# A convolution tap moved to GpSimd in a fused attention and two-layer kernel, with two slots of the first layer moved ahead of the second

## The chip, the cores and the metric

The kernel runs on one core of a Trainium2 chip. The core has five engines, each with its own queue of instructions that runs strictly in order: TensorE (PE in the profile; its weight loads are shown apart as PEld), VectorE (DVE), ScalarE (ACT), GpSimd (POOL) and SyncE (SP), which here only issues DMAs. The engines meet at semaphores. The metric is the device time of one launch in microseconds (us), as the median of several runs.

## The reference

Three stages follow one another for 4 batches of 1088 tokens. Everything is float32.

```
# 1. attention with sketched features, 4 heads of 32
a, b = S1 @ x, S2 @ x                        # r = 8 each
phi(x) = outer(a, b)                         # 64 features
out = (phi(q) @ (phi(k).T @ v)) / (phi(q) @ sum(phi(k)) + 1e-6)

# 2. "layer 1": Fourier mixing, normalisation, an MLP (d_model 128, 512 hidden)
u  = x + real(fft(fft(x, tokens), channels))
un = (u - mean(u)) / sqrt(var(u) + 1e-6)
x2 = u + relu(un @ w_ch1) @ w_ch2

# 3. "layer 2": 1024 hidden channels, a convolution over tokens with 3 taps as gate
h    = relu(x2 @ w_in)
conv = w[0]*h[t-1] + w[1]*h[t] + w[2]*h[t+1]   # per channel
out  = (h * sigmoid(conv)) @ w_out
```

## The kernel before

All operands of a batch pair stay in the core's memory. The order of the work on every engine is written out by hand in one function per engine; nothing schedules it later.

**Attention** (the first 60 us or so) goes batch by batch: `sketches`, `key_values`, `feature_transposes` and `attend` on TensorE, copies out of PSUM on ScalarE, the features and the normalisation on VectorE. SyncE loads keys, queries and values; the queries of a batch come by one DMA (L280).

**Layer 1** is cut into 10 rounds `r` (two batch pairs by five token tiles) of four hidden chunks `c`. One pair (r, c) is a *slot*, numbered n = 4r + c, 0 to 41 (the last two only finish the work). All engines walk the slots in the same order. In a slot TensorE does `up(n)` and `down(n - 2)`. By the chunk, a slot also holds `token_sums(r + 3)` (c = 3) and `normed_transposes(r + 1)` (c = 1) on TensorE; `normed_rows`, `normed_high`, `mixed_high` on ScalarE; `mixed_rows(r + 2)`, `moments(r + 2)` (c = 1), `normed_low(r + 1)` (c = 2) and `mixed_low(r - 1)` on VectorE. The reciprocal standard deviations of a round are eight small instructions of 109x4 elements on GpSimd (L331 to L345), each waiting for the one before; before the change GpSimd does nothing else after its memsets, and they wait for `moments` (L887) alone.

**Layer 2** has 32 steps `i` (4 batches by 8 groups of 128 channels), each of 1088 tokens in three pieces. One step is: `hidden(i, t)` on TensorE (nine matmuls of 128x364, L458 to L460); `relu(i)` on ScalarE (L736, three pieces, into one of 5 buffers `h2`); `middle_tap(i)` on ScalarE (L744, `gate = w[1] * h2` into one of 7 buffers `gate`); `left_tap(i)` and `right_tap(i)` on VectorE (L957 and L962, each `gate += w * shifted h2`, two inputs from SBUF); `sigmoid(i)` on ScalarE (L749); `product(i)` on VectorE (L969, `gate *= h2`, two inputs from SBUF); `project(i)` on TensorE (L540). VectorE's own order in an iteration is `left_tap(i)`, slots, `product(i - 2)`, `right_tap(i)`, slots. ScalarE runs `relu(i + 1)` and `middle_tap(i + 1)`, slots, `sigmoid(i - 1)`.

The first `FIRST_SLOTS` = 22 slots run ahead of layer 2, since its first batches need round 4 finished; the other 20 are spread over the first 15 steps by `slots_a(i)` and `slots_b(i)`. From about step 14 on layer 2 is alone.

Of the kernel before, what the change touches and what calls it, by code (L numbers as in the profile page):

```python
# [89 lines left out]
def build(nc, kT_d, qT_d, v_d, s_d, ident_d, chan_d, cos_d, sin_d, w1_d, w2_d, win_d, wout_d, cw_d, out_d):  # L90
    with ExitStack() as ctx:
# [3 lines left out]
        def sem(name):  # L95
            return ctx.enter_context(nc.semaphore(name))
# [79 lines left out]
        ld_k, ld_q = [[sem(f"ld_{n}{i}") for i in range(2)] for n in "kq"]  # L176
        ld_first, ld_v, ones_ready = sem("ld_first"), sem("ld_v"), sem("ones_ready")
        ld_sketch, ld_ident, ld_tab, ld_w, ld_wout = (sem(n) for n in ("ld_sketch", "ld_ident", "ld_tab", "ld_w", "ld_wout"))
# [35 lines left out]
        def bank_h1(n):  # L214
            return 2 + n % 3 if n < FIRST_SLOTS else 2

# [17 lines left out]
        bank_of = {turn: 3 + n % 2 for n, turn in enumerate(tr_turns)}  # L234
        bank_of.update({turn: 5 + n % 3 for n, turn in enumerate(at_turns)})

        FIRST_SLOTS = NC1 // 2 + 2  # L240
        ALL_SLOTS = NC1 + 2
# [30 lines left out]
        def _(sp):  # L272
            def load_sketched(b):
                if b >= 2:
                    sp.wait_ge(sk_done, 4 * (b - 2) + 4)
                first = KQ_PIECES[0][2] * TK if b == 0 else 0
                if first:
                    sp.dma_start(kT[:, 0, 0:first], kT_d[:, 0, 0:first]).then_inc(ld_first, 16)
                sp.dma_start(kT[:, b % 2, first:], kT_d[:, b, first:]).then_inc(ld_k[b % 2], 16)
                sp.dma_start(qT[:, b % 2], qT_d[:, b, :]).then_inc(ld_q[b % 2], 16)  # L280

# [34 lines left out]
        def _(pool):  # L316
            pool.memset(kvz[:], 0.0).then_inc(kvz_zero, 1)
            pool.memset(half[:], -0.5).then_inc(half_set, 1)
            for x2 in (x2hi, x2lo):
                pool.memset(x2[:, :, 0:1].bitcast(F32), 0.0)  # L320
                pool.memset(x2[:, :, S + 1:SP].bitcast(F32), 0.0).then_inc(zeros_ready, 1)
            pool.wait_ge(half_set, 1)
            for r in range(NR):
                y = rstd[:, r % 2, :]
# [20 lines left out]
                pool.tensor_tensor(shift[:, r % 2, :], negmean, y, ALU.mult).then_inc(rstd_ready, 1)  # L345


        @block.tensor
        def _(pe):
# [10 lines left out]
            def sketches(b, pieces):  # L360

                for side, t0, t1 in pieces:
# [4 lines left out]
                    elif side == 0 and (t0 == 0 or b == 0):  # L367
                        pe.wait_ge(ld_k[b % 2], 16 * (b // 2 + 1))
                    if side == 1 and t0 == 0:
                        pe.wait_ge(ld_q[b % 2], 16 * (b // 2 + 1))  # L370
# [133 lines left out]
            def slot(n):  # L504
                r, c = divmod(n, C1)
                if n < NC1:
                    up(n)
                if 2 <= n < NC1 + 2:
                    down(n - 2)
                if c == 3 and r + 3 < NR:  # L510
                    token_sums(r + 3)
                if c == 1 and r + 1 < NR:
                    normed_transposes(r + 1)
# [53 lines left out]
            for n in range(TR_PIECES):  # L567
                features_and_values(B - 1, n)
                if n == 1:
                    token_sums(0)  # L570
                if n == 3:
                    token_sums(1)
# [12 lines left out]
            for n in range(2, FIRST_SLOTS):  # L585
                slot(n)
# [15 lines left out]
        def _(act):  # L602
# [13 lines left out]
            def feature_copies(b):  # L616
                for n in range(TR_PIECES):
                    act.wait_ge(tr_done, TR_PIECES * b + n + 1)
                    if b >= 1 and n == 0:
                        act.wait_ge(att_done, len(AT_PIECES) * b)  # L620
                    act.activation(qphiT[:, 4 * n:4 * n + 4, :].rearrange("p m t -> p (m t)"),
                                   ps[:, bank_of["features", b, n], 0:4 * TQ], ACT.Copy).then_inc(qphiT_ready, 1)
                    if b == B - 1 and n == 1:
                        sine_copy(0)
# [61 lines left out]
            def slot(n):  # L686
# [7 lines left out]
                if c == 1 and r >= 1:  # L694
                    mixed_high(r - 1)
                if c == 1 and r + 1 < NR:
                    normed_high(r + 1)
# [23 lines left out]
            sine_copy(2)  # L721
            slot(0)
            fold_copies(B - 1)
            slot(1)
            spectrum_copies(B - 1)

# [31 lines left out]

            for n in range(2, FIRST_SLOTS):
                slot(n)  # L760
            relu(0)
            middle_tap(0)
            for n in slots_b(0):
                slot(n)
            for i in range(NI + 1):
                if i + 1 < NI:
                    relu(i + 1)
                    middle_tap(i + 1)
                    for n in slots_b(i + 1):
                        slot(n)  # L770
# [9 lines left out]
        def _(dve):  # L780
# [131 lines left out]
            def slot(n):  # L912
# [38 lines left out]
            slot(0)  # L951
            slot(1)
            partner_fold(B - 1)

# [16 lines left out]

            for n in range(2, FIRST_SLOTS):
                slot(n)
# [108 lines left out]
```

## Time and profile before

| | |
|---|---|
| median of 3 runs | 276.6 us (275.37, 276.6, 279.46) |
| the profiled execution | 278.21 us, of which 276.4 us from the first to the last instruction (the span) |
| mean granted TensorE clock | 0.994 of full speed |
| instructions | 4299 |
| bytes moved by DMA | 13.04 MB |

The profile is of one execution. It has a page of summaries, and its trace answers further questions: the instructions of an engine in order of time (a timeline), groups of instructions of one line and shape with their mean duration, who waited for whom, the chain of work that ended last, and the busy time of each engine in a stretch. Times on a row are the start from the beginning of the span in us and the duration in us, unless ns is written. In square brackets stands the idle time ahead of an instruction, and what ended it. On VectorE and ScalarE an instruction's duration overlaps the next one's by a tenth of a microsecond or so; the distance from start to start is what one costs in a row of them.

### The profile page before, as it was taken

The numbers are of one execution on the slowest core, as the hardware profiler recorded it, in microseconds if no ns is written. First come the engines' busy times: TensorE is split into PE (matmuls) and PEld (weight loads), VectorE is DVE, ScalarE is ACT, GpSimd is POOL, SyncE is SP. The second block draws the span as 40 slices with busy tenths as digits, with TensorE's granted clock in tenths as the row PEclk, the third lists the DMA queues.
The fourth block names the chain that finished last, engine by engine and source line by source line (L and its number), as shares of the span: only waits on it lengthen the run. The fifth ranks groups of instructions, "written<-read, shape, count | busy, mean of one in ns | idle before, by whom it ended". The sixth has DMA issues, their size and how long they took to land.

```text
span 276.4 us, 4299 instructions
## 1 busy us (share of the span) xinstructions
PE 254.7 (92%) x1524; PEld 211.6 (77%) x1524; DVE 219.1 (79%) x384; ACT 186.5 (67%) x353; POOL 36.2 (13%) x90
## 2 busy tenths in 40 slices
PE   8799999989889999979887999999999999999955
PEld 7789999889778888868675777677677777777633
DVE  0746879877887677756686987958699999999993
ACT  2351426234466656648969889796999799999933
POOL 0000000003321233330270740000000000000000
PEclk9999999999999999979999999999999999999999
DMA  6859620200000000000000000000100010001002
GB/s 220 321 209 365 239 90 0 89 4 0 2 0 2 1 1 2 0 1 4 0 0 0 2 0 0 0 4 0 81 0 2 0 81 0 1 4 81 0 0 81
DMA packets 4197, 13.04 MB, mean 47 GB/s; under 512 B 720, under 2 KB 1488, under 8 KB 4176
## 3 DMA queue, kind: packets, MB, share of 16 engines
q1 hardware_dynamic: 4176, 12.77, 12.6%
q8 instruction: 12, 0.20, 0.3%
q14 instruction: 9, 0.07, 0.1%
HBM read 10.54 MB, written 2.23 MB: 46 GB/s over the span
## 4 chain that ended last, share of the span: by engine, by line
PE 45%; DVE 30%; ACT 15%; issue 5%; DMA 2%; POOL 1%; SPq 0%; ACTq 0%; DVEq 0%; POOLq 0%
DVE arena L969 8%; DVE arena L957 8%; DVE arena L962 8%; PE ps L540 7%; PE ps L458 5%; PE ps L451 5%; PE ps L375 5%; ACT arena L662 5%; PE ps L460 4%; PE ps L459 4%; PE ps L416 4%; PE ps L387 4%; ACT arena L749 3%; ACT arena L736 3%; DMA arena<-qT_d 2%
## 5 line engine op out<-in xcount | busy, mean ns | idle before, releaser
L540 PE MATMUL ps<-arena,wout 128*128 128x364 f32 (+1 forms) x192 | 63.8, 471 | 3.5 <-DVE arena L969 3.3
L540 PEld LDWEIGHTS ps<-arena,wout 128*128 128x128 f32 x192 | 35.5, 189 | 21.5 <-DVE arena L969 5.8
L957 DVE SCALAR_TENSOR_TENSOR arena<-arena,taps 128x1088 f32<-128x1088 f32 x32 | 43.5, 1359 | 6.4 <-ACT arena L744 6.4
L458 PE MATMUL ps<-x2hi,wlo 128*128 128x364 f32 x96 | 42.5, 442 | 5.9 <-ACT arena L736 4.2
L736 ACT ACTIVATE arena<-ps 128x364 f32<-128x364 f32 x96 | 40.6, 470 | 10.2 <-PE ps L460 9.9
L962 DVE SCALAR_TENSOR_TENSOR arena<-arena,taps 128x1088 f32<-128x1088 f32 x32 | 43.5, 1358 | 0.0
L969 DVE TENSOR_TENSOR arena<-arena 128x1088 f32<-128x1088 f32 (+2 forms) x36 | 41.8, 1176 | 1.5 <-ACT arena L749 1.5
L744 ACT ACTIVATE arena<-arena,taps 128x1088 f32<-128x1088 f32 x32 | 38.5, 1204 | 1.0
L749 ACT ACTIVATE arena<-arena 128x1088 f32<-128x1088 f32 x32 | 35.2, 1102 | 4.6 <-DVE arena L962 4.6
L460 PE MATMUL ps<-x2hi,whi 128*128 128x364 f32 x96 | 31.8, 332 | 0.0
L459 PE MATMUL ps<-x2lo,whi 128*128 128x364 f32 x96 | 31.7, 330 | 0.0
L458 PEld LDWEIGHTS ps<-x2hi,wlo 128*128 128x128 f32 x96 | 18.2, 189 | 15.1 <-ACT arena L736 9.8
L786 DVE TENSOR_TENSOR arena<-arena 121x2304 f32<-121x2304 f32 (+1 forms) x8 | 21.4, 2690 | 7.4 <-ACT arena L613 7.3
L613 ACT ACTIVATE arena<-ps 109x320 f32<-109x320 f32 (+2 forms) x16 | 6.8, 424 | 22.3 <-PE ps L375 21.2
L459 PEld LDWEIGHTS ps<-x2lo,whi 128*128 128x128 f32 x96 | 18.3, 190 | 4.1 <-issue 1.9
L901 DVE SCALAR_TENSOR_TENSOR h1lo<-ps,h1hi 128x436 fp32r<-128x436 f32 x22 | 13.3, 606 | 9.7 <-ACT h1hi L676 7.8
L331 POOL TENSOR_SCALAR arena<-arena 109x4 f32<-109x4 f32 x10 | 4.0, 401 | 121.5 <-DVE arena L887 121.5
L416 PE MATMUL ps<-arena 128*109 128x66 f32 x160 | 17.5, 261 | 1.3 <-DVE x_nat L826 0.6
L387 PE MATMUL ps<-arena 121*128 121x66 f32 x144 | 18.6, 270 | 0.0
L458 PE MATMUL ps<-unhi,wlo 128*128 128x436 f32 x40 | 17.4, 434 | 1.1 <-ACT arena L633 1.1
L375 PE MATMUL ps<-sketch,arena 128*109 128x64 f32 (+1 forms) x152 | 16.9, 264 | 1.4 <-DMA arena<-qT_d 1.4
L460 PEld LDWEIGHTS ps<-x2hi,whi 128*128 128x128 f32 x96 | 18.2, 190 | 0.0
(81 smaller groups left out, 441.3 us busy)
## 6 DMA issues: line engine op xcount, KB each, us to landing
arena<-v_d SPq DMA_DIRECT2D x4, 594.0 KB, 4.2
arena<-qT_d SPq DMA_DIRECT2D x4, 545.0 KB, 7.0
arena<-kT_d SPq DMA_DIRECT2D x3, 544.5 KB, 7.0
out_d<-arena SPq DMA_DIRECT2D x3, 544.0 KB, 2.7
cos_t<-cos_d SPq DMA_DIRECT2D x1, 926.5 KB, 5.6
sin_t<-sin_d SPq DMA_DIRECT2D x1, 926.5 KB, 7.4
wraw<-w_d SPq DMA_DIRECT2D x2, 256.0 KB, 5.0
wraw<-win_d SPq DMA_DIRECT2D x1, 512.0 KB, 5.9
```

The source lines that it names most:

```text
L375: mm = pe.matmul(ps[0:rows, bank_kq(n), c:c + H * AB], src[:, b % 2, t * rows:(t + 1) * rows], sketch[:], start=True, stop=True)
L387: mm = pe.matmul(ps[:, KV_BANK, pair * 2 * V1:(pair + 1) * 2 * V1], kphi[:, b % 2, t, 2 * pair:2 * pair + 2, :].rearrange("p h f -> p (h f)"),
L458: pe.matmul(out, lo, rhi, start=first, stop=False)
L459: pe.matmul(out, hi, rlo, start=False, stop=False)
L460: return pe.matmul(out, hi, rhi, start=False, stop=last)
L540: pe.matmul(ps[:, OUT_BANK + t, 0:z - a], wout[:, c, :], gate[:, i % GATES, a:z], start=(c == 0), stop=(c == C2 - 1)).then_inc(wout_done, 1)
L736: act.activation(h2[:, i % HIDDENS, t * TT:(t + 1) * TT], ps[:, bank_p(n), 0:TT], ACT.Relu).then_inc(h2_ready, 1)
L744: act.activation(gate[:, i % GATES, 1:S + 1], h2[:, i % HIDDENS, 1:S + 1], ACT.Copy, scale=taps[:, i % C2, 1:2]).then_inc(mid_ready, 1)
L749: act.activation(gate[:, i % GATES, 1:S + 1], gate[:, i % GATES, 1:S + 1], ACT.Sigmoid).then_inc(gate_ready, 1)
L957: dve.scalar_tensor_tensor(out=gate[:, i % GATES, 1:S + 1], in0=h2[:, i % HIDDENS, 0:S], scalar=taps[:, i % C2, 0:1], in1=gate[:, i % GATE ...
L962: dve.scalar_tensor_tensor(out=gate[:, i % GATES, 1:S + 1], in0=h2[:, i % HIDDENS, 2:S + 2], scalar=taps[:, i % C2, 2:3], in1=gate[:, i % ...
L969: dve.tensor_tensor(gate[:, i % GATES, a:z], h2[:, i % HIDDENS, a:z], gate[:, i % GATES, a:z], ALU.mult).then_inc(prod_ready, 1)
```

## The change

`middle_tap` moves from ScalarE to GpSimd, as a `tensor_scalar` with a per-channel multiplier. GpSimd's loop over the rounds is split up so that it walks the slots like the other engines: `reciprocal_deviations(r + 2)` stands in slot c = 1 of round r, behind the middle taps of the steps before it in the queue and ahead of those after it.

Two more slots (22 and 23) run ahead of layer 2: `FIRST_SLOTS` is 24. Around the last batch of attention, slot 1 comes before `fold_transposes(B - 1)` and slot 2 before its spectra; token sums 0 come one piece later; inside a slot, `normed_transposes` and `normed_high` move from c = 1 to c = 2, `normed_low` from c = 2 to c = 3, and the early `mixed_low` from c = 3 to c = 2. The bank of PSUM for two turns changes with it. The first queries are loaded by two DMAs of half the size, and the first query sketches wait for the first of them alone.

The core of the diff:

```diff
-        FIRST_SLOTS = NC1 // 2 + 2
+        FIRST_SLOTS = NC1 // 2 + 4
...
-                sp.dma_start(qT[:, b % 2], qT_d[:, b, :]).then_inc(ld_q[b % 2], 16)
+                part = KQ_PIECES[2][2] * TQ if b == 0 else 0
+                if part:
+                    sp.dma_start(qT[:, 0, 0:part], qT_d[:, 0, 0:part]).then_inc(ld_half, 16)
+                sp.dma_start(qT[:, b % 2, part:], qT_d[:, b, part:]).then_inc(ld_q[b % 2], 16)
...
+            def middle_tap(i):
+                pool.wait_ge(h2_ready, NT * (i + 1))
+                if i >= GATES:
+                    pool.wait_ge(wout_done, NT * (i - GATES + 1))
+                pool.tensor_scalar(gate[:, i % GATES, 1:S + 1], h2[:, i % HIDDENS, 1:S + 1], taps[:, i % C2, 1:2], None,
+                                   ALU.mult).then_inc(mid_ready, 1)
+
+            def slot(n):
+                r, c = divmod(n, C1)
+                if c == 1 and r + 2 < NR:
+                    reciprocal_deviations(r + 2)
+
+            pool.wait_ge(half_set, 1)
+            reciprocal_deviations(0)
+            reciprocal_deviations(1)
+            for n in (*range(FIRST_SLOTS), *slots_a(0), *slots_b(0)):
+                slot(n)
+            pool.wait_ge(ld_wout, 32)
+            for i in range(NI):
+                middle_tap(i)
+                for n in (*slots_a(i + 1), *slots_b(i + 1)):
+                    slot(n)
...
-                if c == 1 and r + 1 < NR:
+                if c == 2 and r + 1 < NR:
                     normed_transposes(r + 1)
...
-                if n == 1:
+                if n == 2:
                     token_sums(0)
...
             slot(0)
+            slot(1)
             fold_transposes(B - 1)
-            slot(1)
+            slot(2)
             channel_spectra(B - 1)
...
-            def middle_tap(i):
-                act.wait_ge(h2_ready, NT * (i + 1))
-                if i == 0:
-                    act.wait_ge(ld_wout, 32)
-                if i >= GATES:
-                    act.wait_ge(wout_done, NT * (i - GATES + 1))
-                act.activation(gate[:, i % GATES, 1:S + 1], h2[:, i % HIDDENS, 1:S + 1], ACT.Copy,
-                               scale=taps[:, i % C2, 1:2]).then_inc(mid_ready, 1)
...
-                if c == 2 and r + 1 < NR:
+                if c == 2 and 1 <= r < NJ:
+                    mixed_low(r - 1)
+                if c == 3 and r + 1 < NR:
                     normed_low(r + 1)
-                if c == 3 and 1 <= r < NJ:
-                    mixed_low(r - 1)
```

On GpSimd the end of the queue before is the last of ten such groups of eight:

```order
L331 TENSOR_SCALAR arena<-arena 109x4
L333 TENSOR_TENSOR arena<-arena,half 109x4
L334 TENSOR_SCALAR arena<-arena 109x4
L337 TENSOR_TENSOR arena<-arena 109x4
L339 TENSOR_TENSOR arena<-arena 109x4
L341 TENSOR_SCALAR arena<-arena 109x4
L343 TENSOR_TENSOR arena<-arena 109x4
L345 TENSOR_TENSOR arena<-arena 109x4
```

On GpSimd the end of the queue in the change, from the last instruction of round 8's group (L350) on; L356 is the middle tap, and the group between is round 9's:

```order
L350 TENSOR_TENSOR arena<-arena 109x4
L356 TENSOR_SCALAR arena<-arena,taps 128x1088 x4
L336 TENSOR_SCALAR arena<-arena 109x4
L338 TENSOR_TENSOR arena<-arena,half 109x4
L339 TENSOR_SCALAR arena<-arena 109x4
L342 TENSOR_TENSOR arena<-arena 109x4
L344 TENSOR_TENSOR arena<-arena 109x4
L346 TENSOR_SCALAR arena<-arena 109x4
L348 TENSOR_TENSOR arena<-arena 109x4
L350 TENSOR_TENSOR arena<-arena 109x4
L356 TENSOR_SCALAR arena<-arena,taps 128x1088 x28
```

So all of round 8's group now stands ahead of the first middle tap, and round 9's between the fourth and the fifth.

On VectorE before, where layer 2 begins (L957 left tap, L962 right tap; L866 and L872 `mixed_rows`, L881 and L887 `moments`, L894 `normed_low`, L908 `mixed_low`):

```order
L887 BN_AGGR arena<-arena 109x2 x4
L894 TENSOR_TENSOR unlo<-ps,unhi 128x436
L957 SCALAR_TENSOR_TENSOR arena<-arena,taps 128x1088
L962 SCALAR_TENSOR_TENSOR arena<-arena,taps 128x1088
L866 TENSOR_TENSOR arena<-ps,arena 109x130 x2
L872 TENSOR_TENSOR arena<-x_nat,arena 109x2x64 x4
L957 SCALAR_TENSOR_TENSOR arena<-arena,taps 128x1088
L908 TENSOR_TENSOR x2lo<-ps,x2hi 128x2x109
L908 TENSOR_TENSOR x2lo<-ps,x2hi 128x2x108
L881 BN_STATS arena<-arena 109x6 x4
L887 BN_AGGR arena<-arena 109x2 x4
```

On VectorE in the change, the same place (L979 left tap, L984 right tap; L887 and L893 `mixed_rows`, L902 and L908 `moments`, L915 `normed_low`, L929 `mixed_low`):

```order
L915 TENSOR_TENSOR unlo<-ps,unhi 128x436
L887 TENSOR_TENSOR arena<-ps,arena 109x130 x2
L893 TENSOR_TENSOR arena<-x_nat,arena 109x2x64 x4
L929 TENSOR_TENSOR x2lo<-ps,x2hi 128x2x109
L929 TENSOR_TENSOR x2lo<-ps,x2hi 128x2x108
L902 BN_STATS arena<-arena 109x6 x4
L908 BN_AGGR arena<-arena 109x2 x4
L979 SCALAR_TENSOR_TENSOR arena<-arena,taps 128x1088
L984 SCALAR_TENSOR_TENSOR arena<-arena,taps 128x1088
L979 SCALAR_TENSOR_TENSOR arena<-arena,taps 128x1088
L984 SCALAR_TENSOR_TENSOR arena<-arena,taps 128x1088
```

`mixed_rows(8)`, a `mixed_low` and `moments(8)` have moved from behind the first left tap to ahead of it.

## Rows read from the trace of the kernel before

**Rows 1.** The page, busy time and share of the span by engine.

```profile
PE 254.7 (92%) x1524; PEld 211.6 (77%) x1524; DVE 219.1 (79%) x384; ACT 186.5 (67%) x353; POOL 36.2 (13%) x90
```

**Rows 2.** Windows of all engines: stretch, length, busy us (instructions) each, PE clock, DMA.

```profile
126.46:201.79 75.33, 70.80 (x324) 52.31 (x323) 60.21 (x81) 64.67 (x118) 15.87 (x16) 1.00 0.02 8
201.79:265.29 63.50, 61.56 (x265) 46.73 (x266) 63.50 (x53) 58.60 (x90) 0.00 (x0) 1.00 0.05 18
260.00:264.00 4.00, 2.31 (x8) 1.06 (x6) 4.00 (x5) 3.34 (x6) 0.00 (x0) 1.00 0.00 0
120.00:122.00 2.00, 2.00 (x8) 1.95 (x7) 1.01 (x6) 0.94 (x2) 1.28 (x3) 0.54 0.00 0
```

**Rows 3.** The chain of work that ended last, in order of time: start, us, what.

```profile
98.74 1.33 PE ps L451 x12
...
106.21 1.33 PE ps L451 x12
...
265.29 1.26 DVE arena L957
266.56 1.21 DVE arena L969
267.81 5.79 PE ps L540 x18
```

**Rows 4.** Timeline of VectorE, 126 to 163 us.

```profile
126.46 1.35 DVE L957 SCALAR_TENSOR_TENSOR arena<-arena,taps 128x1088 f32<-128x1088 f32 x1 [5.42 <-ACT arena L744]
...
158.41 1.34 DVE L962 SCALAR_TENSOR_TENSOR arena<-arena,taps 128x1088 f32<-128x1088 f32 x1
159.67 1.34 DVE L957 SCALAR_TENSOR_TENSOR arena<-arena,taps 128x1088 f32<-128x1088 f32 x1
160.93 1.28 DVE L969 TENSOR_TENSOR arena<-arena 128x1088 f32<-128x1088 f32 x1
162.13 1.35 DVE L962 SCALAR_TENSOR_TENSOR arena<-arena,taps 128x1088 f32<-128x1088 f32 x1
```

**Rows 5.** Timeline of GpSimd, 60 to 170 us: an undisturbed group's ends, then one in layer 2.

```profile
112.58 0.20 POOL L331 TENSOR_SCALAR arena<-arena 109x4 f32<-109x4 f32 x1 [4.64 <-DVE arena L887]
...
115.20 0.20 POOL L345 TENSOR_TENSOR arena<-arena 109x4 f32<-109x4 f32 x1
...
153.15 1.14 POOL L331 TENSOR_SCALAR arena<-arena 109x4 f32<-109x4 f32 x1 [9.31 <-DVE arena L887]
...
158.62 1.19 POOL L343 TENSOR_TENSOR arena<-arena 109x4 f32<-109x4 f32 x1
159.89 2.39 POOL L345 TENSOR_TENSOR arena<-arena 109x4 f32<-109x4 f32 x1
```

**Rows 6.** Groups by line and shape, whole span: count | busy us, mean ns | idle before.

```profile
L744 ACT ACTIVATE arena<-arena,taps 128x1088 f32<-128x1088 f32 x32 | 38.5, 1204 | 1.0
L317 POOL MEMSET arena<- 128x132 f32 x1 | 0.2, 208 | 0.3 <-POOLq L1074 0.3
L320 POOL MEMSET x2hi<- 128x4 f32 x1 | 0.1, 105 | 0.0
```

**Rows 7.** Waits: who for whom, us in total, times, longest us.

```profile
DVE x2lo L908 <- ACT x2hi L682: 12.5, 5, 3.0
PE ps L471 <- ACT arena L662: 2.4, 6, 0.5
PE ps L375 <- DMA arena<-qT_d: 1.4, 1, 1.4
PE ps L458 <- DVE x2lo L908: 1.4, 1, 1.4
```

**Rows 8.** Timeline of TensorE and ScalarE where layer 2 begins.

```profile
119.71 0.41 PE L458 MATMUL ps<-x2hi,wlo 128*128 128x364 f32 x1 [1.36 <-DVE x2lo L908]
...
125.14 1.21 ACT L744 ACTIVATE arena<-arena,taps 128x1088 f32<-128x1088 f32 x1
```

More of the change, by code:

```diff
@@ L176, in build @@
         ld_k, ld_q = [[sem(f"ld_{n}{i}") for i in range(2)] for n in "kq"]
-        ld_first, ld_v, ones_ready = sem("ld_first"), sem("ld_v"), sem("ones_ready")
+        ld_first, ld_half, ld_v, ones_ready = (sem(n) for n in ("ld_first", "ld_half", "ld_v", "ones_ready"))
         ld_sketch, ld_ident, ld_tab, ld_w, ld_wout = (sem(n) for n in ("ld_sketch", "ld_ident", "ld_tab", "ld_w", "ld_wout"))
@@ L214, in bank_h1 @@
         def bank_h1(n):
-            return 2 + n % 3 if n < FIRST_SLOTS else 2
+            return 2 + n % 3 if n < NC1 // 2 + 2 else 2
         def bank_x2(r):
@@ L235, in build @@
         bank_of.update({turn: 5 + n % 3 for n, turn in enumerate(at_turns)})
-        FIRST_SLOTS = NC1 // 2 + 2
+        for n in range(2):
+            bank_of["folded", B - 1, n] = bank_of["spectra", B - 1, n] = (5, 7)[n]
+        FIRST_SLOTS = NC1 // 2 + 4
         ALL_SLOTS = NC1 + 2
@@ L321, in _, with reciprocal_deviations @@
                 pool.memset(x2[:, :, S + 1:SP].bitcast(F32), 0.0).then_inc(zeros_ready, 1)
-            pool.wait_ge(half_set, 1)
-            for r in range(NR):
+            def reciprocal_deviations(r):
                 y = rstd[:, r % 2, :]
@@ L368, in sketches @@
                         pe.wait_ge(ld_k[b % 2], 16 * (b // 2 + 1))
-                    if side == 1 and t0 == 0:
+                    if side == 1 and t0 == 0 and b == 0:
+                        pe.wait_ge(ld_half, 16)
+                    elif side == 1:
                         pe.wait_ge(ld_q[b % 2], 16 * (b // 2 + 1))
@@ L581, in _ @@
             slot(0)
+            slot(1)
             fold_transposes(B - 1)
-            slot(1)
+            slot(2)
             channel_spectra(B - 1)
-            for n in range(2, FIRST_SLOTS):
+            for n in range(3, FIRST_SLOTS):
                 slot(n)
@@ L622, in feature_copies @@
                                    ps[:, bank_of["features", b, n], 0:4 * TQ], ACT.Copy).then_inc(qphiT_ready, 1)
-                    if b == B - 1 and n == 1:
+                    if b == B - 1 and n == 2:
                         sine_copy(0)
@@ L695, in slot @@
                     mixed_high(r - 1)
-                if c == 1 and r + 1 < NR:
+                if c == 2 and r + 1 < NR:
                     normed_high(r + 1)
@@ L722, in _ @@
             slot(0)
+            slot(1)
             fold_copies(B - 1)
-            slot(1)
+            slot(2)
             spectrum_copies(B - 1)
@@ L757, in output @@
                     act.activation(outT[:, b % 2, a:z], ps[:, OUT_BANK + t, 0:z - a], ACT.Copy).then_inc(out_ready, 1)
-            for n in range(2, FIRST_SLOTS):
+            for n in range(3, FIRST_SLOTS):
                 slot(n)
             relu(0)
-            middle_tap(0)
             for n in slots_b(0):
@@ L767, in _ @@
                     relu(i + 1)
-                    middle_tap(i + 1)
                     for n in slots_b(i + 1):
@@ L952, in _ @@
             slot(1)
+            slot(2)
             partner_fold(B - 1)
@@ L970, in product @@
                                       ALU.mult).then_inc(prod_ready, 1)
-            for n in range(2, FIRST_SLOTS):
+            for n in range(3, FIRST_SLOTS):
                 slot(n)
```

## The prediction

> **What bounds the kernel now.** I read the busy shares first, then the chain of waits, then windows cut at the steps of layer 2. The page alone misleads: TensorE is busy 92% of the span and VectorE 79% [rows 1], which looks like a kernel bound by TensorE. The windows say where each engine limits. Between left taps 14 and 31 (201.79 to 265.29 us) VectorE is busy 63.50 of 63.50 us [rows 2]: 17 steps at 63.50 / 17 = 3.735 us. That is 1.26 us from start to start of a left tap, 1.20 of a product, 1.26 of a right tap [rows 4], and nothing between them. ScalarE is busy 58.60 us there and does not set the pace [rows 2]. Between left taps 0 and 14 (126.46 to 201.79 us), where 20 slots of layer 1 are mixed in, VectorE is busy 60.21 of 75.33 us and TensorE 70.80 [rows 2]; of VectorE's 15.1 us of idle time most is the five waits of `mixed_low` for ScalarE, 12.5 us [rows 7], behind TensorE's slots. The rest of the span after left tap 31 is 276.4 - 265.29 = 11.1 us of product, projection and store [rows 3].
>
> So layer 2 is VectorE's own chain for its second half and close to it in the first. The middle tap costs ScalarE 32 x 1.204 us = 38.5 us [rows 6], and none of that is on VectorE's path in the second half. Taking it from ScalarE can give back something only in the first half, or before it.
>
> **GpSimd beside VectorE.** The question is what a GpSimd instruction of 1088 columns does beside VectorE's taps. The trace has no such instruction, but it has small ones in both surroundings. Round 7's group of eight, with VectorE on PSUM work or idle, runs from 112.58 to 115.40 us, 2.8 us, single instructions at 0.20 us [rows 5]. Round 9's begins at 153.15 and ends at 162.28 us, 9.1 us for the same eight [rows 5]. Its members last until a tap or product of VectorE ends: L343 ends at 159.81, right tap L962 at 159.75; L345 starts at 159.89, lasts through left tap L957 (to 161.01) and product L969 (to 162.21), and ends at 162.28 [rows 4, 5]. So a GpSimd instruction does not run while VectorE runs an instruction with two inputs from SBUF, and once it even missed the change-over. The Trainium skill ("SBUF — State Buffer", who interferes with whom) has this as a rule: the two engines share a pair of ports, held by one of them for a whole instruction, and a VectorE instruction with two SBUF inputs needs it against a GpSimd one that reads SBUF. The trace agrees as far as GpSimd waiting for VectorE goes; that VectorE waits for GpSimd in turn no row shows, since 0.2 us fits into a change-over (VectorE's starts keep their 1.26 us) [rows 4]. All three VectorE instructions of a step are of the kind that kept GpSimd out, and they fill the engine. A long GpSimd instruction therefore must either hold VectorE off, or wait until VectorE runs dry for want of the next middle tap. Either way the two take turns.
>
> **How long the tap is on GpSimd.** The lower bound: two memsets, 132 columns in 208 ns and 4 in 105 ns, give 103 / 128 = 0.80 ns a column [rows 6]; with 0.20 us for a small instruction [rows 5], 0.20 + 1084 x 0.80 = 1.07 us. The upper bound: reading and writing cost that slope each, 0.20 + 1084 x 1.61 = 1.94 us. I take 1.1 us, since the memset is the only row with a slope and ScalarE does the same thing in 1.20 [rows 6]. The Trainium skill ("GPSIMD Engine Reference", engine selection) puts one-input elementwise work on GpSimd at roughly line rate, and advises VectorE for such work; no run here has shown it yet, and the sum would be the same by it.
>
> **The sum,** against the execution's own span of 276.4 us.
>
> 1. *Second half of layer 2.* In turns, a step costs 3.735 + 1.1 + about 0.1 for the hand-over and the semaphore = 4.95 us. 17 x (4.95 - 3.735) = +20.7 us. The path is then left tap, product, right tap, middle tap of the next step. ScalarE (less its 1.2 us a step) and TensorE, busy at most 61.56 / 17 = 3.6 us a step, are clear of it [rows 2].
> 2. *First half.* VectorE's busy 60.21 us [rows 2] lose some 3.6 us, as one `mixed_rows`, one `mixed_low` and one `moments` now stand ahead of left tap 0: 56.6. Fourteen middle taps at 1.2 us add 16.8: 73.4. Round 9's group stands between middle taps 3 and 4: VectorE gets no left tap 4 until the group (2.8 us undisturbed, longer beside product 1 and right tap 3) and then the tap are through, about 3 us of VectorE idle. Of the 15.1 us of idle time before, most was VectorE waiting for TensorE's slots; a slower VectorE lets TensorE run ahead, so I keep 5. Together 81.5 us instead of 75.3: +6.2.
> 3. *Before left tap 0.* Two more slots at (106.21 - 98.74) / 4 = 1.87 us each [rows 3]: +3.7 until TensorE's first `hidden`, at 119.71 us before [rows 8]. Filled by them or by the new order: the 1.36 us wait in front of it [rows 8], most of the 2.4 us of L471 [rows 7], most of the 1.4 us for the first queries [rows 7], and a little around the last fold; I take 4.4, so `hidden(0)` starts near 119.0. From there left tap 0 took 126.46 - 119.71 = 6.75 us. Now TensorE does two and a bit more slots (4.2 us, to the down product of slot 23), ScalarE `mixed_high` (0.7), VectorE `mixed_low` and `moments` (2.0), GpSimd round 8's group (2.8) and middle tap 0 (1.1), one behind the other: 10.8, to about 129.9 us. +3.4. Bounds: -4 if the group were not in the way, +6.
> 4. *The end.* The product and projection of the last steps have no middle tap beside them: 0.
> 5. *Clock.* At 120 to 122 us the granted clock was 0.54 (near the 1.2 GHz level) after TensorE's wait in front of layer 2 [rows 2, 8]; that may go, worth about 1 us, and lies inside item 3's margin.
>
> Sum: 276.4 + 20.7 + 6.2 + 3.4 = 306.7 us of span. The profiled execution took 278.21 us with 1.8 us outside the span, and was 1.6 us above the median of 276.6; so the span plus 0.2 is the median: 307 us.
>
> **The rivals.**
>
> A. *In turns at about 1.1 us (the forecast).* 307 us; its own range 297 to 317, from items 2 and 3.
>
> B. *In turns, but the tap is slow on GpSimd,* up to 1.94 us: 0.84 us more in each of 31 steps, +26, so 333 us. Against it stands only ScalarE's time for the same thing. Beyond 1.94 us no row gives a bound; I leave it a little chance.
>
> C. *The hold is finer than an instruction,* so that GpSimd uses the port in VectorE's gaps. A tap of 1088 columns leaves little: the VectorE chain has perhaps 0.1 us per instruction in which nothing streams (the overlap of 1.35 us durations at 1.26 us spacing [rows 4]), 0.3 us a step. Then a step costs 3.735 + 0.8: 276.4 + 17 x 0.8 + 3 + 3 = 296 us, or 288 where the rest hides too. For it: VectorE's starts show no delay from small GpSimd instructions. Against it: GpSimd's waits are of whole instructions.
>
> D. *No cost to VectorE: faster.* GpSimd waits at most at its start and then streams beside VectorE. The second half keeps 63.5 us, the first half falls to VectorE's 56.6 us plus 10 of idle time, and left tap 0 comes at about 127: 127 + 66.6 + 63.5 + 11.1 = 268 us. It decides if GpSimd's 1.1 us costs VectorE less than about 0.1 us a step. The 2.39 us that a 0.20 us instruction needed speaks against it; a tap that only waits at its start would still leave VectorE whole.
>
> E. *TensorE turns slow.* It would be idle a third of each step, and at 1.2 GHz its 3.6 us a step would be about 6, above 4.95: 17 x 1 more, 325 us. Against it: from 260 to 264 us it was busy 2.31 of 4 us at a granted clock of 1.00 [rows 2].
>
> **How the numbers follow.** A 0.60, B 0.12, C 0.12, D 0.10, E and what I have not thought of 0.06. The prediction is A's 307. The range takes A, C, and the lower half of B: 288 to 328. Faster or slower by over 2% is about what a measurement of this kernel can tell from no change. Slower takes A, B, C and E: 0.88. The same (271 to 282) is D with less in the first half, or C with nearly all hidden: 0.05. Faster is D: 0.07.
>
> **What would show it.** In the profile after, GpSimd's L356 should come 32 times, with durations well over 1.1 us where they wait for VectorE. VectorE's left taps (L979) should start 4.95 us apart in the second half, each waiting for POOL L356 about 1.2 us, and the chain of waits should name L356 in about a fifth of the span. ScalarE should fall by 38 us of busy time without any gain. Left tap 0 should start near 130 us, with round 8's group and a middle tap in front of it. I am wrong if VectorE's taps keep 3.74 us from start to start (D), if the step is 4.5 us or less (C), or if it is above 5.5 (B or E; then the duration of L356 with VectorE idle, or the granted clock, tells which).

## The result and the profile after

The changed kernel takes 319.14 us (median of 4 runs, 314.8 to 319.9), the kernel before 277.5 us beside it (275.37 to 279.46). The ratio is 1.145, with a 95% interval of 1.129 to 1.161: slower. The time lies within the predicted range of 288 to 328 us, 12 us above the predicted 307.

One thing is needed to read the single numbers: the executions of one kernel differ by how long TensorE's granted clock stayed at its lower level, here 314.8 us at a mean clock of 0.956 and 318.85 us at 0.935, and a ratio is of the faster executions of both kernels alone, while a median is of all. The profiled one is the 314.8 us, with a span of 313.0.

The page of the changed kernel, busy time by engine and the costliest group:

```profile
PE 265.0 (85%) x1524; PEld 218.0 (70%) x1524; DVE 241.8 (77%) x384; ACT 153.6 (49%) x321; POOL 146.1 (47%) x122
...
L356 POOL TENSOR_SCALAR arena<-arena,taps 128x1088 f32<-128x1088 f32 x32 | 119.4, 3737 | 38.4 <-ACT arena L768 38.3
```

Against [rows 1], ScalarE lost 33 us of busy time, GpSimd gained 110, and VectorE gained 22.7 though it runs the same 384 instructions. Windows of the changed kernel, cut at left taps 0, 14 and 31 as in [rows 2] (columns as there):

```profile
135.56:221.47 85.91, 66.42 (x282) 50.31 (x282) 65.04 (x65) 43.66 (x86) 56.20 (x23) 0.90 0.02 7
221.47:299.80 78.33, 62.25 (x258) 44.53 (x257) 78.33 (x52) 40.20 (x71) 64.33 (x17) 1.00 0.04 15
299.80:313.00 13.20, 9.74 (x22) 5.05 (x20) 6.52 (x10) 3.64 (x5) 0.00 (x0) 0.75 0.12 42
```

| stretch, us of the span | before | forecast | after | difference |
|---|---|---|---|---|
| to left tap 0 | 126.5 | 129.9 | 135.6 | +9.1 |
| left tap 0 to 14 | 75.3 | 81.5 | 85.9 | +10.6 |
| left tap 14 to 31 | 63.5 | 84.2 | 78.3 | +14.8 |
| left tap 31 to the end | 11.1 | 11.1 | 13.2 | +2.1 |
| span | 276.4 | 306.7 | 313.0 | +36.6 |

**The second half of layer 2.** Timelines of VectorE and GpSimd in the changed kernel. L984 is the right tap, L979 the left tap, L991 the product, L356 GpSimd's middle tap:

```profile
238.71 1.34 DVE L984 SCALAR_TENSOR_TENSOR arena<-arena,taps 128x1088 f32<-128x1088 f32 x1
239.97 2.17 DVE L979 SCALAR_TENSOR_TENSOR arena<-arena,taps 128x1088 f32<-128x1088 f32 x1
242.07 1.28 DVE L991 TENSOR_TENSOR arena<-arena 128x1088 f32<-128x1088 f32 x1
...
238.64 4.23 POOL L356 TENSOR_SCALAR arena<-arena,taps 128x1088 f32<-128x1088 f32 x1 [1.60 <-ACT arena L768]
```

GpSimd starts at 238.64, is kept out by the right tap until about 240.0, and then the left tap takes 2.17 instead of 1.34 us. After that VectorE goes on while GpSimd still works until 242.87. VectorE is busy 78.33 of 78.33 us: it never waits for a middle tap here. What it pays is one instruction for each middle tap that is 0.8 to 0.9 us longer (17 in 17 steps, though some steps have two and the next none), and (78.33 - 63.50) / 17 = 0.87 us a step.

**The first half** has real waits. The changed kernel, first VectorE, then TensorE (L481 are token sums, L488 the up product of round 8):

```profile
135.56 2.17 DVE L979 SCALAR_TENSOR_TENSOR arena<-arena,taps 128x1088 f32<-128x1088 f32 x1 [6.06 <-POOL arena L356]
...
142.61 0.60 DVE L915 TENSOR_TENSOR unlo<-ps,unhi 128x436 fp32r<-128x436 f32 x1
...
166.99 2.26 DVE L979 SCALAR_TENSOR_TENSOR arena<-arena,taps 128x1088 f32<-128x1088 f32 x1 [5.46 <-POOL arena L356]
...
143.36 2.48 PE L481 MATMUL ps<-folded,cos_t 109*109 109x130 f32 x10 [9.31 <-DVE unlo L915]
...
173.25 0.70 PE L488 MATMUL ps<-unhi,wlo 128*128 128x436 f32 x1 [7.56 <-issue]
```

and the waits of the same kernel, whole span:

```profile
DVE arena L979 <- POOL arena L356: 20.6, 8, 6.1
PE ps L481 <- DVE unlo L915: 9.5, 2, 9.3
```

VectorE waited 20.6 us for middle taps, all of it in front of and in the first half. TensorE waited 9.3 and 7.6 us for `normed_low`, which is queued on VectorE behind left and right taps (the token sums need it because they share a bank of PSUM with the transposes that it reads). The granted clock fell while TensorE stood still and stayed down for some microseconds behind each stop. It was 0.54 in the mean from 143 to 150 us and 0.50 from 170 to 175, two more rows of windows:

```profile
143.00:150.00 7.00, 6.64 (x29) 6.66 (x30) 3.03 (x9) 1.87 (x4) 0.00 (x0) 0.54 0.00 0
170.00:175.00 5.00, 1.75 (x4) 1.50 (x5) 5.00 (x5) 0.28 (x1) 3.35 (x1) 0.50 0.01 3
```

**In front of layer 2.** TensorE reached the first `hidden` later, not earlier (119.71 before [rows 8]), and the first middle tap took 3.06 us on an undisturbed GpSimd:

```profile
122.37 0.41 PE L488 MATMUL ps<-x2hi,wlo 128*128 128x364 f32 x1
...
132.39 3.06 POOL L356 TENSOR_SCALAR arena<-arena,taps 128x1088 f32<-128x1088 f32 x1
```

### The profile page after: what moved, and what is told of

Its sections match the earlier page's. It is cut to its first block, busy times and chain, and to the rows that moved or that the text cites. A ratio compares the mean times of both kernels' runs of the same rounds, so it can differ in the third digit from the quotient of the medians.

```text
span 313.0 us, 4304 instructions
## 1 busy us (share of the span) xinstructions
PE 265.0 (85%) x1524; PEld 218.0 (70%) x1524; DVE 241.8 (77%) x384; ACT 153.6 (49%) x321; POOL 146.1 (47%) x122
## 3 DMA queue, kind: packets, MB, share of 16 engines
q1 hardware_dynamic: 4320, 12.77, 11.2%
## 4 chain that ended last, share of the span: by engine, by line
PE 46%; DVE 31%; issue 9%; POOL 7%; ACT 6%; POOLq 0%; DVEq 0%; ACTq 0%
DVE arena L979 10%; DVE arena L984 9%; DVE arena L991 8%; PE ps L570 7%; POOL arena L356 5%; PE ps L488 5%; PE ps L405 5%; PE ps L490 4%; PE ps L489 4%; PE ps L417 4%; PE ps L481 4%; PE ps L446 4%; PE ps L531 2%; PE ps L430 2%; ACT arena L693 2%
## 5 line engine op out<-in xcount | busy, mean ns | idle before, releaser
L356 POOL TENSOR_SCALAR arena<-arena,taps 128x1088 f32<-128x1088 f32 x32 | 119.4, 3737 | 38.4 <-ACT arena L768 38.3
L570 PE MATMUL ps<-arena,wout 128*128 128x364 f32 (+1 forms) x192 | 67.9, 493 | 16.1 <-DVE arena L991 15.2
L979 DVE SCALAR_TENSOR_TENSOR arena<-arena,taps 128x1088 f32<-128x1088 f32 x32 | 53.3, 1666 | 20.7 <-POOL arena L356 20.6
L570 PEld LDWEIGHTS ps<-arena,wout 128*128 128x128 f32 x192 | 36.2, 197 | 38.7 <-DVE arena L991 22.4
L336 POOL TENSOR_SCALAR arena<-arena 109x4 f32<-109x4 f32 x10 | 2.9, 291 | 109.0 <-DVE arena L908 109.0
L984 DVE SCALAR_TENSOR_TENSOR arena<-arena,taps 128x1088 f32<-128x1088 f32 x32 | 53.7, 1678 | 0.1
L488 PE MATMUL ps<-x2hi,wlo 128*128 128x364 f32 x96 | 44.1, 459 | 4.3 <-ACT arena L768 4.1
L768 ACT ACTIVATE arena<-ps 128x364 f32<-128x364 f32 x96 | 41.7, 471 | 9.6 <-PE ps L490 9.1
L991 DVE TENSOR_TENSOR arena<-arena 128x1088 f32<-128x1088 f32 (+2 forms) x36 | 42.9, 1203 | 0.0
L488 PEld LDWEIGHTS ps<-x2hi,wlo 128*128 128x128 f32 x96 | 18.6, 194 | 13.0 <-ACT arena L768 8.3
L488 PE MATMUL ps<-unhi,wlo 128*128 128x436 f32 x40 | 17.0, 426 | 10.0 <-issue 8.5
L707 ACT ACTIVATE arena<-ps 128x436 f32<-128x436 f32 x18 | 9.7, 537 | 20.3 <-PE ps L490 19.3
L922 DVE SCALAR_TENSOR_TENSOR h1lo<-ps,h1hi 128x436 fp32r<-128x436 f32 x22 | 13.2, 602 | 8.1 <-ACT h1hi L707 8.1
L481 PE MATMUL ps<-folded,cos_t 109*109 109x130 f32 x68 | 10.5, 300 | 9.5 <-DVE unlo L915 9.5
```

Of the source, the lines that this page charges most:

```text
L356: pool.tensor_scalar(gate[:, i % GATES, 1:S + 1], h2[:, i % HIDDENS, 1:S + 1], taps[:, i % C2, 1:2], None, ALU.mult).then_inc(mid_ready, 1)
L488: pe.matmul(out, lo, rhi, start=first, stop=False)
L570: pe.matmul(ps[:, OUT_BANK + t, 0:z - a], wout[:, c, :], gate[:, i % GATES, a:z], start=(c == 0), stop=(c == C2 - 1)).then_inc(wout_done, 1)
L768: act.activation(h2[:, i % HIDDENS, t * TT:(t + 1) * TT], ps[:, bank_p(n), 0:TT], ACT.Relu).then_inc(h2_ready, 1)
L979: dve.scalar_tensor_tensor(out=gate[:, i % GATES, 1:S + 1], in0=h2[:, i % HIDDENS, 0:S], scalar=taps[:, i % C2, 0:1], in1=gate[:, i % GATE ...
L984: dve.scalar_tensor_tensor(out=gate[:, i % GATES, 1:S + 1], in0=h2[:, i % HIDDENS, 2:S + 2], scalar=taps[:, i % C2, 2:3], in1=gate[:, i % ...
```

## The experiments

The diffs are shortened: indices, waits and semaphores are partly left out, and the comments are mine.

### Taking the change apart

**e1: the tap alone on GpSimd, all else as before.**

```diff
-            relu(0)
-            middle_tap(0)
+            relu(0)
...
+            for i in range(NI):
+                middle_tap(i)              # on GpSimd, as in the change
+                for n in (*slots_a(i + 1), *slots_b(i + 1)):
+                    slot(n)
```

> The kernel before with the middle tap on GpSimd alone; the order of layer 1, the two moved slots and the halved load of queries stay as before. Theory (the tap causes the whole loss: VectorE is held off 0.92 us a step, and a tap of 3.04 us on GpSimd starves it in the mixed half): near the changed kernel, 305 to 320 us, with left taps 4.6 us apart in the second half. Rival (the new order of the slots causes the loss of the first half, 22 us of 37): about 276.6 + 15 = 292 us.

Measured: 305.4 and 306.1 us at a mean granted clock of 0.977, 313.7 and 314.5 us at 0.951, the median 309.9; ratio 1.107 (1.094 to 1.119). Its windows, between the same left taps (0 at 128.76 us):

```profile
128.76:213.91 85.15, 72.16 (x322) 54.40 (x321) 67.56 (x81) 49.12 (x102) 59.38 (x31) 0.96 0.02 7
213.91:293.13 79.22, 63.41 (x258) 45.42 (x257) 78.45 (x52) 40.18 (x71) 65.38 (x17) 0.98 0.04 15
```

The tap alone makes the losses of both halves (+9.8 and +15.7 us) and 2.3 us in front of them: 28 of the 37. The 2.3 us are the least sure part. The tap itself is 1.9 us longer (3.06 after 1.21), but `hidden(0)` also came 1.9 us later in this execution (121.57), and the stretch at a clock of 0.54 that followed it before [rows 2] is not there.

**e2: all but the tap.** The changed kernel with `middle_tap` back on ScalarE.

```diff
             for i in range(NI):
-                middle_tap(i)              # GpSimd
...
             relu(0)
+            middle_tap(0)                  # ScalarE, as before
...
                     relu(i + 1)
+                    middle_tap(i + 1)
```

> The changed kernel with the middle tap back on ScalarE; the two moved slots, the new order and the halved load stay. Theory (the tap is the whole loss, the rest fills waits): 272 to 276 us, 1 to 4 us under the kernel before, with left tap 0 at 127 to 129 us. Rival (the new order delays normed_low on VectorE and costs TensorE time by itself): 285 to 300 us, with TensorE waiting over 5 us for L915's counterpart.

Measured: 285.2 us, ratio 1.032 (1.025 to 1.039). Both expectations missed something. The rest costs 3.2%, where the theory saw a gain. That is in the rival's range, but not through `normed_low`: TensorE waits for it 1.6 us in all. Left tap 0 comes at 130.8 us, +4.3. The second half is 63.4 us as before, the first 78.1 (+2.8). In that half TensorE has one stop of 4.2 us, and behind it the clock is at half. The rows are of e2's ScalarE (L684 is `normed_rows`), TensorE and windows:

```profile
130.80:208.92 78.12, 67.12 (x296) 49.58 (x294) 57.46 (x67) 60.65 (x105) 17.88 (x16) 0.96 0.02 8
...
161.20 1.65 ACT L684 ACTIVATE arena<-arena 109x128 f32<-109x128 f32 x4 [2.33 <-POOL arena L350]
...
164.26 0.67 PE L479 MATMUL ps<-x2hi,wlo 128*128 128x364 f32 x1 [4.23 <-ACT arena L759]
...
164.00:170.00 6.00, 5.74 (x12) 4.08 (x13) 2.44 (x2) 2.24 (x4) 0.00 (x0) 0.50 0.00 0
```

ScalarE waits for round 9's group on GpSimd, which lasts from 149.51 to 161.17 us beside VectorE's taps (compare [rows 5]), and TensorE stops until ScalarE has emptied its banks. Before, ScalarE waited for that group only 0.7 us. That group and its reader have come closer together. The two slots alone did not do it: with them alone (e11 below) ScalarE waits 0.8 us for it and TensorE never more than 1.8 us for the rectified pieces. Which part of the new order does it was not separated.

**e6: the new order and the halved load, without the two slots and the tap.**

```diff
-        FIRST_SLOTS = NC1 // 2 + 4
+        FIRST_SLOTS = NC1 // 2 + 2
```

> The changed kernel with the tap on ScalarE and with 22 slots ahead of layer 2: only the new order and the halved load of queries are left of the change. e2 lost 7 us without the tap. Theory (the order is neutral, since rounds came 7.42 us apart in e2 and 7.47 us before, and the two slots are the loss: they put off layer 2 by 2 x 1.87 us, which VectorE's chain pays in full at the end): 275 to 278 us. Rival (the order is the loss): 281 to 285 us.

Measured: 281.8 us, ratio 1.012 (1.002 to 1.022). That is in the rival's range; the order costs about 1%, or 3 us beside the 278.5 of the kernel before, and is not neutral.

**e11: the two slots alone.**

```diff
-        FIRST_SLOTS = NC1 // 2 + 2
+        FIRST_SLOTS = NC1 // 2 + 4
```

> The kernel before with 24 instead of 22 slots ahead of layer 2 and nothing else changed; the tap stays on ScalarE. e2 (all but the tap) took 285.2 us and e6 (the same with 22 slots) 281.8. Theory (the two slots cost 3.4 us by themselves and the rest of the new order 3): 279 to 281 us. Rival (only together do they cost, since order and slots meet in front of layer 2): 276 to 278 us.

Measured: 281.8 us, ratio 1.010 (1.004 to 1.015), just above what the theory had; the slots do cost by themselves. Slots 1.0% and order 1.2% are 2.2%; e2 has both and loses 3.2%. The difference lies within the intervals of the three ratios, so that the two cost more together than apart is not shown.

**e12: the halved load alone** (the diff of the change's `load_sketched` and `sketches`, on the kernel before).

> The kernel before with the first queries loaded by two DMAs of half the size and nothing else changed. Theory (TensorE's 1.4 us wait for the queries goes, but VectorE's query features, which need both halves, come no sooner): 276 to 277.5 us. Rival (it moves all that follows forward by the wait): 275 to 275.5 us. A second rival (one more DMA among the first delays the loads behind it): 279 to 280 us, which would be e6's loss.

Measured: 278.45 us beside 278.55, ratio 1.000 (0.997 to 1.004). By the ratio that is the theory, though both numbers lie above its 277.5. TensorE's sketches now run without the gap of [rows 7], and nothing comes of it:

```profile
5.38 6.85 PE L380 MATMUL ps<-sketch,arena 128*121 128x64 f32 x66
...
7.85 7.76 DVE L791 TENSOR_TENSOR arena<-arena 121x2304 f32<-121x2304 f32 x3 [6.73 <-ACT arena L618]
```

VectorE's features (L791) follow one another for 7.8 us. They end at 15.61 us after 16.25 before, so they did come a little sooner; in this execution that is lost again by layer 2 (left tap 0 at 127.17 us), with a granted clock of 0.84 from 70 to 80 us where it had been 1.00.

**e3: ScalarE's taps for steps 0 to 13, GpSimd's for 14 to 31.**

```diff
+                if i == 14:
+                    pool.wait_ge(mid_ready, 14)
+                if i >= 14:
+                    middle_tap(i)          # GpSimd
...
+                    if i + 1 < 14:
+                        middle_tap(i + 1)  # ScalarE
```

> The changed kernel with the middle taps of steps 0 to 13 on ScalarE and those of steps 14 to 31 on GpSimd. Theory (two separate costs: 0.92 us of VectorE held off in each step wherever GpSimd makes the tap, and the starved VectorE only in the mixed half): e2 plus 17 x 0.87 = +15 us plus up to 3 us for the hand-over at step 14, so 288 to 293 us, left taps 4.6 us apart from step 14 on. Rival (the loss of the second half is a late effect of the first, since the engines come in out of step): under e2 + 6 us.

The number was reckoned from e2 at 273 us and missed; from e2 as measured, the theory gives 300 to 303 us. One execution took 301.7 us at a mean clock of 0.982, and all are far above the rival's e2 + 6 us: the cost of the second half does not need the first. The three others took 307.6 to 308.2 us at 0.949 to 0.954, and the profile is of one of those (window from left tap 14 to 31, and one left tap in it):

```profile
210.71:294.17 83.46, 66.52 (x256) 48.24 (x256) 76.97 (x52) 40.06 (x71) 66.95 (x17) 0.91 0.03 14
...
273.57 2.26 DVE L994 SCALAR_TENSOR_TENSOR arena<-arena,taps 128x1088 f32<-128x1088 f32 x1 [2.86 <-POOL arena L356]
```

Here VectorE was not always busy, and the granted clock fell in the stretch itself: 83.5 us instead of 78.3. In such an execution VectorE does wait for middle taps, 2.86 us at a time. Ahead of this wait TensorE stood still for 2.7 us, its next projection took 3.8 us instead of 2.0 at a clock of 0.56 (261 to 264 us), and GpSimd idled 3.0 us for the pieces of `relu` before it could start a tap at 267.00. The forecast's rival E is this, as an addition to the main effect in some executions.

### What GpSimd does to VectorE

**e4: a probe.** The kernel before, with one GpSimd instruction more in each of steps 14 to 31, three of each of six kinds, on which nothing waits.

```diff
+            for i in range(14, NI):
+                pool.wait_ge(h2_ready, NT * (i + 1))
+                kind = (i - 14) // 3
+                if kind == 0:
+                    pool.tensor_scalar(scratch[:], wraw[:, 0:1088], taps[:, 0, 1:2], None, ALU.mult)
...
+                elif kind == 2:
+                    pool.memset(scratch[:], 0.5)
```

> The kernel before with one more GpSimd instruction in each of steps 14 to 31, from constant data into a scratch tensor that nobody reads, so nothing waits for it: three each of a multiply by a per-channel operand over 1088 columns, one by an immediate over 1088, a memset of 1088, the multiply by operand over 544, a copy of 1088, and a multiply of two tensors of 1088. Theory (GpSimd keeps VectorE off only while it reads, about 1088 columns at 1.2 GHz = 0.9 us): one VectorE instruction in each step is 0.9 us longer for both multiplies and the copy, 0.45 for 544 columns, 0 for the memset, more than 0.9 for two inputs; 276.6 + 3 x (0.9 + 0.9 + 0 + 0.45 + 0.9 + 1.8) = about 291 us. Rival (the hold lasts the whole instruction and only looked shorter because VectorE was waiting anyway): about 3 us for each multiply, and the memset holds too.

Measured: 290.6 and 295.3 us against about 291 forecast, the first the profiled one. VectorE's and GpSimd's rows of e4, one for each kind that differs (L358 the multiply by a per-channel operand, L362 the memset, L364 the 544 columns, L366 the copy, L368 two inputs):

```profile
202.57 2.17 DVE L985 SCALAR_TENSOR_TENSOR arena<-arena,taps 128x1088 f32<-128x1088 f32 x1
204.67 1.34 DVE L980 SCALAR_TENSOR_TENSOR arena<-arena,taps 128x1088 f32<-128x1088 f32 x1
...
221.72 1.33 DVE L985 SCALAR_TENSOR_TENSOR arena<-arena,taps 128x1088 f32<-128x1088 f32 x1
...
234.17 1.72 DVE L980 SCALAR_TENSOR_TENSOR arena<-arena,taps 128x1088 f32<-128x1088 f32 x1
...
249.94 2.18 DVE L985 SCALAR_TENSOR_TENSOR arena<-arena,taps 128x1088 f32<-128x1088 f32 x1
...
259.06 3.08 DVE L985 SCALAR_TENSOR_TENSOR arena<-arena,taps 128x1088 f32<-128x1088 f32 x1
```

```profile
201.11 4.37 POOL L358 TENSOR_SCALAR scratch<-wraw,taps 128x1088 f32<-128x1088 f32 x1 [0.17 <-POOL scratch L358]
221.62 1.00 POOL L362 MEMSET scratch<- 128x1088 f32 x1 [1.56 <-ACT arena L759]
232.84 2.84 POOL L364 TENSOR_SCALAR scratch<-wraw,taps 128x544 f32<-128x544 f32 x1 [2.47 <-ACT arena L759]
249.66 1.31 POOL L366 COPY scratch<-wraw 128x1088 f32<-128x1088 f32 x1 [1.99 <-ACT arena L759]
258.82 2.18 POOL L368 TENSOR_TENSOR scratch<-wraw 128x1088 f32<-128x1088 f32 x1 [2.03 <-ACT arena L759]
```

Against 1.34 us undisturbed, VectorE's instruction is longer by 0.83 us for the multiply and the copy (up to 0.92 at other places), as much for the multiply by an immediate (3.2 us long), 0.38 for 544 columns, 1.74 for two inputs of 1088, and not at all for the memset. So the price goes by the columns that GpSimd reads, 0.8 to 0.9 us for 1088, and not by how long its instruction lasts or, as far as the memset shows, by what it writes. The whole-instruction rival falls.

**e7: a copy instead of the multiply,** in the changed kernel. It leaves out the middle tap's weight.

```diff
-                pool.tensor_scalar(gate[...], h2[...], taps[:, i % C2, 1:2], None, ALU.mult)
+                pool.tensor_copy(gate[...], h2[...])
```

> The changed kernel with a plain copy in place of the multiply on GpSimd (the middle tap's weight is left out, so the gate differs from the reference). A copy held VectorE off as long as the multiply in e4, 0.9 us, but was over in 1.3 instead of 3.0 us. Theory (the second half is paid by the hold, the first half by the length of the instruction): second half 78 us as in the changed kernel, left tap 0 about 2 us earlier, first half 79 to 82 instead of 85.9 us, in all 303 to 309 us. Rival (the hold makes the whole loss): unchanged, 315 us or more.

Measured: 306.2 us, ratio 1.101 (1.087 to 1.114). Windows from left tap 0 to 14 and on to 31:

```profile
134.56:215.29 80.73, 65.56 (x279) 49.69 (x278) 63.95 (x66) 43.73 (x87) 23.82 (x22) 0.92 0.02 7
215.29:292.95 77.66, 64.43 (x259) 46.12 (x259) 77.66 (x53) 40.22 (x72) 27.00 (x17) 0.97 0.04 15
```

The copies lasted 1.13 us at the median (1.09 at the least) instead of 3.53. The second half stayed (77.7 us after 78.3), the first fell by 5.2 us. That is the theory; only left tap 0 came 1.0 and not 2 us earlier, as the first copy started 1.0 us later (133.35) than the first multiply (132.39).

**e8: a memset instead of the multiply.** It leaves out the middle tap.

```diff
+                pool.memset(gate[...], 0.1)
```

> The changed kernel with a memset of the same 1088 columns in place of the multiply on GpSimd (the middle tap is left out of the computation). It reads nothing, and in e4 it held VectorE off by nothing. Theory (what costs is GpSimd's read of SBUF): second half back to 63.5 us, in all as e2 or a little under it, 280 to 286 us. Rival (moving the step to a third engine costs semaphore time by itself): 290 us or more.

Measured: 286.8 us, 0.8 above the theory's range, ratio 1.031 (1.018 to 1.044), e2's 1.032 again.

```profile
133.39:210.63 77.24, 65.78 (x275) 49.77 (x274) 57.48 (x66) 43.32 (x86) 17.99 (x22) 0.91 0.02 8
210.63:274.02 63.39, 61.34 (x265) 46.36 (x265) 63.39 (x52) 43.57 (x73) 17.10 (x17) 1.00 0.05 18
```

With nothing read, VectorE's second half is 63.39 us again. Moving a step to a third engine costs nothing by itself there; GpSimd's read does.

### The first half's stops, and a better kernel

**e9: `normed_low` of rounds 7 to 9 one slot earlier,** in the changed kernel.

```diff
-                if c == 3 and r + 1 < NR:
+                if c == (3 if r < 6 else 2) and r + 1 < NR:
                     normed_low(r + 1)
```

> The changed kernel with normed_low of rounds 7 to 9 one slot earlier on VectorE, as before the change. TensorE stood still for 9.3 and 7.6 us until VectorE had done normed_low (L915), which was queued behind left and right taps that waited for GpSimd. Theory (that queueing makes much of the first half's loss): the first stall 5 us shorter, first half 79 to 83 instead of 85.9 us, in all 308 to 315 us. Rival (VectorE, waiting for GpSimd's taps, sets the first half, and TensorE's stalls are only its shadow): within 2 us of the changed kernel, 317 to 320 us.

Measured: 315.1 us, between the two expectations, ratio 1.131 (1.120 to 1.143), beside the changed kernel's 1.145 (1.129 to 1.161): not told apart. TensorE's first stop fell from 9.3 to 5.75 us, but the first half only from 85.9 to 84.5:

```profile
139.74 2.48 PE L481 MATMUL ps<-folded,cos_t 109*109 109x130 f32 x10 [5.75 <-DVE unlo L915]
...
220.02:303.81 83.79, 65.84 (x245) 46.97 (x245) 75.20 (x53) 40.79 (x71) 64.84 (x17) 0.89 0.03 14
```

So the stops look to be mostly the shadow of VectorE's waits: this stop is 3.6 us shorter and the half only 1.4. In this profile the second half took 83.8 us at a granted clock of 0.89, and VectorE waited three times 2.9 us for middle taps in it, as in e3.

**e10: no middle tap at all.** The outer taps are divided by the middle one once; the sigmoid scales by it.

```diff
-                dve.wait_ge(mid_ready, i + 1)
-                dve.scalar_tensor_tensor(out=gate, in0=h2[..., 0:S], scalar=taps[:, i % C2, 0:1], in1=gate, ...)
+                dve.wait_ge(h2_ready, NT * (i + 1))
+                dve.scalar_tensor_tensor(out=gate, in0=h2[..., 0:S], scalar=ratio[:, i % C2, 0:1], in1=h2[..., 1:S + 1], ...)
...
-                act.activation(gate, gate, ACT.Sigmoid)
+                act.activation(gate, gate, ACT.Sigmoid, scale=taps[:, i % C2, 1:2])
```

> The kernel before without any middle tap: the outer taps are divided by the middle one once on VectorE (two multiplies and a reciprocal of 128x8), left_tap adds h itself instead of what middle_tap wrote, and the sigmoid on ScalarE scales by the middle tap. The result is the same function. VectorE's three instructions of a step stay at 3.73 us. Theory (the tap lies off VectorE's chain in the second half, and ScalarE's 38 us are worth something only where VectorE waits for ScalarE or TensorE, in front of layer 2 and in its first half): second half 63.4 us as before, left tap 0 1 to 2 us earlier, first half 72 to 75 us: 272 to 275 us. Rival (TensorE's 70.8 us of work in the first half bound it, and the earlier start is lost again): 276 to 277 us.

Measured: ratio 0.994 (0.990 to 0.998), median 276.6 us beside 278.55. It is 0.6% faster than the kernel before, and so than the changed one; this is less than the theory's 1 to 2%, and the number is the rival's. Taking 38 us of work off ScalarE, at next to no cost to another engine, is worth about 2 us (1 to 3 by the interval). With the order of the kernel before, moving the tap could hardly have earned more. Its profile is of an execution of 308 us, with a mean granted clock of 0.58 in its first 60 us, so where the gain arises stays open.

## Why the prediction came out as it did

**Right: the direction, and where the cost arises.** The second half is VectorE's chain, what ScalarE gives up is not on it, and GpSimd's tap takes time from VectorE's two-input instructions. e8 against e7 and the changed kernel shows the last, and e10 how little was to be had. The turns for a whole instruction, on which the number rested, are not what happens.

**Step 1, the second half, +20.7 forecast, +14.8 measured.** I let the two engines take turns for the whole instruction and put 1.1 + 0.1 us on it. GpSimd keeps VectorE out only as long as its reads account for (e4), 0.87 us a step; the rest of its 3 us runs beside VectorE. The step took 78.33 / 17 = 4.61 us, between the 4.95 forecast and the 4.5 that was to show rival C. C had the hold finer than an instruction, and that part of it is right, with 0.8 us a step; but it got its 0.8 from a tap of 1.1 us less VectorE's gaps, and the hold goes by columns read. That my number came near is luck: two errors met here. With the tap's real 3.04 us, whole-instruction turns would have given 17 x (3.04 + 0.1) = 53 us. The sign "each left tap waits for L356 about 1.2 us" was wrong: VectorE is busy 78.33 of 78.33 us, and its own instruction is longer. ScalarE fell by 33 us of busy time and not 38, and L356 has 5% of the chain and not a fifth. The Trainium skill ("SBUF — State Buffer", SBUF: two separate sides) says that whoever starts first gets the shared ports for the whole instruction, and the other fully blocks. For VectorE holding GpSimd off the trace agrees ([rows 5] and L356's 4.23 us). For GpSimd holding VectorE off it does not: 0.8 to 0.9 us out of 3.0.

**How long the tap is: 1.1 us forecast, bound 1.94, measured 3.06.** This was the weakest step. The memset's slope is right for a memset (1.00 us for 1088 columns in e4) and close for a copy (1.09), and says nothing of a multiply. The upper bound rested on the same slope twice, so it bounded nothing. Rival B had the direction, but priced the length in all 31 steps; it counts only where VectorE runs dry.

**Step 2, the first half, +6.2 forecast, +10.6 measured.** The group between taps 3 and 4 did what was said: left tap 4 comes at 166.99 us, 11 us after left tap 3, with 5.5 us of VectorE idle where I had about 3. The size was off by the length of the tap: with the copy of e7 the half takes 80.7 us, against 81.5 forecast.

**Step 3, before left tap 0, +3.4 forecast, +9.1 measured.** Two terms failed. I let the two slots fill 4.4 us of waits, and `hidden(0)` came at 122.4 instead of 119.0. The slots' 3.7 us were paid with 1.0 us won. The waits of L471 vanished [rows 7], but rounds still came 7.42 us apart after 7.47, and the halved load gained nothing (e12). A wait that goes is a gain only if nothing else is as late; I had costed each by its length. Not all of it is the order: from 70 to 80 us the granted clock was 0.83 here and 1.00 before. Of the rest, 2.0 us are the tap, 3.06 for 1.1 us, and 0.4 the chain ahead of it.

**Step 4, the end, 0 forecast, +2.1 measured.** The last projection ran at a granted clock of 0.75 [the window above]; in e1, e2, e7 and e8 the end takes 11.2 us, about as before.

**The rest of the change, 3.7 us less 4.4 before `hidden(0)` in the forecast,** is a loss of 3.2% by itself (e2). Two errors in sum 3 and the length of the tap worked upwards, the hold downwards, and they partly cancelled: 306.7 against 313.0 us of span. The median lies another 4.3 us above the profiled execution; the others had a mean clock of 0.935 for its 0.956. Where in the span they lost it no trace shows; e3 and e9 show one such place, the second half.

## What to carry to other kernels

Before moving a step to GpSimd, look at what VectorE does at that time. If it is the bound and runs instructions with two inputs from SBUF, what GpSimd reads there is paid on the critical path, here 0.8 to 0.9 us for 1088 float32 columns, however idle GpSimd is; a memset, which only writes, cost nothing. And take the work off an engine only if that engine is on the path: here 38 us of ScalarE's work were worth about 2 us even when they were simply left out.

Waits ahead of a stage are not a sum that can be filled. Price a moved block by when its successor starts, with its full length as the default.

## What the runs showed of the hardware

- A GpSimd instruction that reads 1088 float32 columns makes one two-input VectorE instruction beside it 0.83 to 0.92 us longer, 544 columns 0.38 to 0.46, two inputs of 1088 1.74. A memset does nothing to it (e4, e8).
- GpSimd, 128 partitions by 1088 columns of float32: a memset 1.00 us (e4), a copy 1.09 at the least (e7), a multiply by a per-channel operand 3.04 at the least (the changed kernel), a multiply of two tensors 2.0 to 2.2 (e4). The two-tensor multiply is shorter than the one by an operand. The Trainium skill ("GPSIMD Engine Reference", engine selection) calls one-input work roughly line rate. The copy agrees, at 1.09 us beside the 1.2 to 1.3 of one of VectorE's two-input instructions of that size; the multiply by an operand does not.
- TensorE, idle for about a fifth of the stretch (busy 62.25 of 78.33 us), kept its clock in one execution and lost it in others: 78.3 us at 1.00 in the changed kernel, 83.8 at 0.89 in e9, 83.5 at 0.91 in e3, for the same stretch.
